# Attention and two feed-forward layers on one core: raw keys and queries of two heads transposed side by side, reciprocals spread through DRAM, a written order per tile

## The reference

```
def _attn_ref(q, k, v):                       # q, k, v: 4 x 8 heads x 1152 x 64
    q_pool = q.reshape(B, H, S // 2, 2, D).mean(axis=3)
    scores = scale * np.matmul(q_pool, k.transpose(0, 1, 3, 2))
    scores = scores - np.max(scores, axis=-1, keepdims=True)
    attn = np.exp(scores)
    attn = attn / (np.sum(attn, axis=-1, keepdims=True) + 1e-09)
    return np.matmul(attn, v)

# x = attention's output as 2304 tokens x 512
h = x @ w_in                                  # 512 x 2048
x = np.where(h >= 1, h, np.where(h <= -1, 0, (h + 1) ** 2 / 4)) @ w_out
x = np.maximum(np.maximum(x @ w1, x @ w2), x @ w3) @ w2_out      # 512 x 768, 768 x 512
```

## Time and profile before

| | us |
|---|---|
| runs | 1294.75, 1292.39, 1293.17 |
| median | 1293.17 |
| the profiled execution's own time | 1294.91 |
| its span, first to last instruction | 1293.0 |
| PE busy in the span | 1259.6 (97%) |
| DVE, ACT, POOL busy | 758.1, 658.8, 335.5 |

### The profile page before, as it was taken

One profiled execution on the slowest core, in us unless ns is written; L12 is line 12 of the kernel. 1 busy time (PEld: TensorE's weight loads), 2 busy tenths in 40 slices (PEclk: granted clock), 3 DMA queues, 4 the chain that ended last, 5 costly groups with the idle time before them and its releaser, 6 DMA issues.

```text
span 1293.0 us, 21136 instructions
## 1 busy us (share of the span) xinstructions
PE 1259.6 (97%) x7876; PEld 1207.9 (93%) x7876; DVE 758.1 (59%) x1579; ACT 658.8 (51%) x1570; POOL 335.5 (26%) x332
## 2 busy tenths in 40 slices
PE   7999999999999999989999999999999999999998
PEld 6989899999989898979999999999999999999997
DVE  5888888888888888874544444444453222223221
ACT  5989899999989898962222222222222111111111
POOL 5343443444433444258600000000282000000000
PEclk9999999999999999989999999999999999999999
DMA  3111111111111111113300000000030000000000
GB/s 119 47 56 56 52 33 57 53 41 56 56 47 56 56 56 38 52 49 100 113 1 1 1 1 1 1 1 1 17 122 26 1 25 25 1 25 5 20 25 25
DMA packets 59140, 49.07 MB, mean 38 GB/s; under 512 B 2977, under 2 KB 48033, under 8 KB 59041
## 3 DMA queue, kind: packets, MB, share of 16 engines
q1 hardware_dynamic: 59040, 47.72, 12.1%
HBM read 42.99 MB, written 4.72 MB: 37 GB/s over the span
## 4 chain that ended last, share of the span: by engine, by line
PE 79%; ACT 18%; DVE 1%; issue 1%; POOL 1%; DMA 0%; SPq 0%; POOLq 0%; ACTq 0%
PE hid L868 33%; PE acc L900 16%; ACT probs L558 8%; PE trans L413 8%; ACT pT_hi L548 6%; PE acc L932 6%; PE scores L456 6%; PE values L475 5%; PE scores L458 4%; ACT kT L568 1%; ACT value_aux L582 1%; PE trans L424 1%; DVE qT L662 1%; ACT X L578 1%; ACT qT L571 1%
## 5 line engine op out<-in xcount | busy, mean ns | idle before, releaser
L626 DVE TENSOR_REDUCE neg_max_parts<-scores 128x1 f32<-128x384 f32 x432 | 234.7, 552 | 44.0 <-PE scores L458 30.3
L548 ACT ACTIVATE pT_hi<-trans 128x384 fp32r<-128x384 f32 x432 | 191.2, 491 | 55.8 <-PE trans L413 52.3
L640 DVE TENSOR_TENSOR pT_lo<-trans,pT_hi 128x384 fp32r<-128x384 f32 x432 | 212.0, 546 | 7.3 <-ACT pT_hi L548 6.3
L558 ACT ACTIVATE probs<-scores,neg_max 128x768 f32<-128x768 f32 (+1 forms) x288 | 212.0, 753 | 4.0 <-DVE neg_max L633 4.0
L456 PE MATMUL scores<-kT,qT 128*128 128x384 f32 x480 | 199.6, 416 | 9.4 <-ACT probs L558 9.1
L413 PE MATMUL trans<-ident,probs 128*128 128x128 f32 x1296 | 189.7, 273 | 9.6 <-DVE qT L662 6.4
L413 PEld LDWEIGHTS trans<-ident,probs 128*128 128x128 f32 x1296 | 157.5, 140 | 24.9 <-DVE qT L662 11.5
L868 PE MATMUL hid<-qT,w_slots 128*128 128x384 f32 x936 | 171.6, 336 | 0.0
L868 PE MATMUL hid<-x_hi,w_slots 128*128 128x384 f32 x624 | 167.6, 335 | 0.0
L868 PEld LDWEIGHTS hid<-qT,w_slots 128*128 128x128 f32 x936 | 163.7, 188 | 1.0
L986 ACT ACTIVATE excess<-rise,halves 128x384 f32<-128x384 f32 x96 | 59.2, 617 | 203.0 <-DVE rise L1070 203.0
(11 more groups left out here) (101 smaller groups left out, 1998.2 us busy)
## 6 DMA issues: line engine op xcount, KB each, us to landing
k_raw<-in_k SPq DMA_DIRECT2D x16, 576.0 KB, 4.0
v_raw<-in_v SPq DMA_DIRECT2D x32, 288.0 KB, 2.8
q_raw<-in_q SPq DMA_DIRECT2D x32, 256.0 KB, 3.0
out<-X SPq DMA_DIRECT2D x18, 256.0 KB, 2.8
q_raw<-in_moe_w_out SPq DMA_DIRECT2D x14, 256.0 KB, 3.1
k_raw<-in_moe_w SPq DMA_DIRECT2D x12, 256.0 KB, 3.1
k_raw<-in_moe_w_in SPq DMA_DIRECT2D x8, 256.0 KB, 2.9
k_raw<-in_moe_w_out SPq DMA_DIRECT2D x8, 256.0 KB, 3.0
```

The costliest lines, as they stand in the source:

```text
L548: act.activation(*tile_places(pT[0], src, t, g), ACT.Copy).then_inc(p_hi_done, 1)
L558: act.activation(probs[:, par, :].rearrange("p (n k) -> p n k", n=GROUPS)[:, ns[0]:ns[-1] + 1], scores[:, bank:bank + len(ns), 0:SB], ACT. ...
L626: dve.tensor_reduce(neg_max_parts[:, par, n:n + 1], scores[:, score_banks(u9)[n], 0:SB], AX_X, ALU.max, negate=True).then_inc(parts_done, 1)
L640: dve.tensor_tensor(*tile_places(pT[1], src, t, g), hi.bitcast(F32), ALU.subtract).then_inc(p_lo_done, 1)
```

## The change

Keys: `load_k` writes two heads side by side (runs of 64 elements), PE transposes the raw keys, 9 blocks in three groups, ACT writes the high part (`k_hi_done`), DVE the remainder (`k_lo_done`), both into `k_parts`, and SP places them in `kT` with four copies of 64 partitions. Queries: POOL adds the neighbours so that two heads stand side by side, PE transposes 4 blocks and one for the shared tile, ACT and DVE write `q_parts`, SP places them with eight copies. Values: ACT keeps a whole block with one instruction, SP moves the other head's half under its partner (`move_values`), POOL adds. Reciprocals: SP writes the 128x9 to DRAM (4-byte runs), reads them back with three broadcasts into `recip_cols`, and POOL multiplies all of a pair's `X` (`scale`). The first pair keeps the old layout; its keys are split by DVE as before, after both new loads. The order strings now differ from tile to tile. At the end POOL splits eight weight chunks early, the high part of the first `X` tile is written by ACT, and no transposes of reciprocals stand between the first products.

```
-PREP = {0: [("K", 0)], 1: [("K", 1)], 2: [("K", 2)], 3: [("K", 3)], 4: [("K", 4), ("R", 0)],
-        5: [("K", 5)], 6: [("R", 1), ("Q", 0), ("Q", 1), ("Q", 2)]}
-PE_ORDER = ["S1", "T0", "S2", "T1", "T2", "N0", "V", "X"]
-ACT_ORDER = ["T0", "T1", "T2", "E0", "E1", "X", "V"]
-DVE_ORDER = ["T0", "T1", "T2", "M0", "X", "M1", "M2"]
+PE_ORDER = """
+S1.1 S1.2
+T0.0 T0.1 S2.0 W2:10-14 K0 T0.2 W2:14-18 S2.1 S2.2
+T1.0 T1.1 T1.2 S3.0 W3:0-4 W3:4-8 K1 S3.1 W3:8-10 S3.2
+T2.0 T2.1 S4.0 T2.2 K2 S4.1
+T3.0 S4.2 T3.1 W3:10-13 S5.0 T3.2 W3:13-15 Q0 S5.1 W3:15-18
+T4.0 S5.2 T4.1 V0:0-4 S6.0 T4.2 V0:4-8 S6.1 S6.2
+T5.0 Q1 V0:8-13 S7.0 V0:13-18 T5.1 S7.1 S7.2 T5.2
+T6.0 S8.0 T6.1 V1:0-4 T6.2 V1:4-8 S8.1 S8.2
+T7.0 T7.1 V1:8-13 T7.2 V1:13-18
+T8.0 S9.0 S9.1 S9.2 T8.1 T8.2 S10.0 V2:0-5 V2:5-10
+"""
...
-    KG, QG, RG = 6, 3, 2
+    KG, QG = 3, 2
...
-            sp.dma_start(k_raw, k_heads[bass.ds(head(pair), 2)].rearrange("h p n -> p h n")
-                         ).then_inc(k_loaded, 16)
+            for h in range(2):
+                src = k_heads[bass.ds(head(pair) + h, 1)].rearrange("h p (t d) -> p (h t) d", d=D)
+                sp.dma_start(k_raw[:, :, h, :], src).then_inc(k_loaded, 16)
...
+        def place_k(pair):
+
+            sp.wait_ge(k_lo_done, pair * KG)
+            for h in range(2):
+                for a in range(2):
+                    copy_parts(sp, kT[rows_of(a), pair % 2, h, :], k_parts[rows_of(h), a, :], k_placed)
+
+        def place_q(pair):
+
+            sp.wait_ge(q_lo_done, (pair - 1) * QG + 1)
+            for part, dst in enumerate((qT_hi, qT_lo)):
+                for h in range(2):
+                    at = (2 + 4 * h) * P
+                    for copy in range(2):
+                        copy_parts(sp, dst[rows_of(copy), pair % 2, at:at + 4 * P], q_parts[rows_of(h), part, :], q_placed)
...
+        def scale(pair):
+
+            pool.wait_ge(recip_spread, 48 * (pair + 1))
...
+            x = X[:, bass.ds(pair * SQ, SQ)]
+            pool.tensor_tensor(x, x, recip_cols[:], ALU.mult).then_inc(scaled, 1)
...
-    EARLY = 3
+    EARLY, EARLY_LOADS = 8, 5
...
+        if n == 0:
+            pool.wait_ge(*ends["keys_placed"])
+        elif n == 1:
+            pool.wait_ge(*ends["scores_done"])
+        elif n == 2:
+            pool.wait_ge(*ends["values_done"])
+        split_weights(pool, n, n)
```

More of the change, by code:

```diff
@@ L144, in prep_of, with ring_order @@
-    def prep_of(u, t, first, last):
-        return [(kind, g) for kind, g in PREP.get(t, [])
-                if not (kind == "R" and first and u == 0) and not (kind in "KQ" and last and u == 1)]
-    def group_count(kind, pair, t, g):
+    WARM_UP, BRIDGE = 22, 10
+    FIRST = [("FK", 0), ("FK", 1), ("FK", 2), ("FQ", 0)]
+    SECOND = [("FK", 3), ("FK", 4), ("FK", 5), ("FQ", 1), ("FQ", 2)]
+    def ring_order():
+        groups = FIRST + SECOND
+        for pair in range(PAIRS):
+            for step in steps_of(PE_ORDER):
+                if step[0] == "T":
+                    groups.append(("T", pair * TILES + step[1], step[2]))
+                elif step[0] in "KQ" and pair + 1 < PAIRS:
+                    groups.append((step[0], pair + 1, step[1]))
+        return groups
@@ L289, in sp_program @@
[L289 to L316 removed]
+        load_v(0, 0)
@@ L437, in tile_scores @@
[L437 to L443 removed]
+                last = pe.transpose(trans[:, BANK[group], j * P:(j + 1) * P], probs[:, s % 2, at:at + P], ident[:])
+            last.then_inc(tile_trans_done, 1)
@@ L874, in hidden1 @@
         idx = tile * C1 + f
+        if idx == 0:
+            pe.wait_ge(*ends["exp_done"])
         if f == 0:
@@ L942, in two_tiles1 @@
                 for f in range(C1):
-                    if not (first and u == 0 and f < EARLY):
-                        hidden1(pe, tile, f, u)
+                    hidden1(pe, tile, f, u)
                     if f >= LAG1:
```

955 lines of the change are left out of this document (478 added, 477 removed).

## The result

The changed kernel takes 1311.7 us (median of 4 runs, 1308.6 to 1315.6), the kernel before 1292.85 beside it: a ratio of 1.0145, interval 1.0132 to 1.0159. It is slower where 1250 was forecast. The profiled execution has a span of 1313.9 us against 1293.0. From the page of the changed kernel: the span, busy time of PE, granted clock and DMA share in forty slices, packets, and the load queue.

What follows compares the result with a forecast made beforehand. PE was taken as the bound, ACT and DVE close behind. From 1294.9 us, 40.3 off for 15.5 attention pairs at 32.2 us, 2 added at the start, 6 off at attention's end: 1250.6, stated as 1250, range 1231 to 1271.

Runs made afterwards that it cites:

- e1: The changed kernel with the reciprocals stored as 128 runs of 36 bytes instead of 1152 single 4-byte numbers (output wrongly scaled): 1271.96 us.
- e4: The changed kernel with the reciprocals transposed by PE, copied by ACT and stored as 9 runs of 512 bytes behind the second move: 1277.02 us.
- e5: e4 with SP's next keys' load moved from behind the keys' copies to behind the queries' copies: 1270.01 us.
- e2: The changed kernel with SP issuing the eight queries' copies right behind the four keys' copies, scattered store kept: 1324.76 us.
- e8: The changed kernel with the same scattered store of reciprocals issued by ACT into its own DMA queue instead of by SP: 1332.65 us.
- e9: The changed kernel with the scattered store issued behind the values' load and second move, and at the end a move right behind it: 1319.31 us.

## What to carry to other kernels

Price every transfer that a change adds by how its writes lie in DRAM, not by its bytes: a scattered store of touching 4-byte numbers cost 40 us (the changed kernel against e1), and one small transpose ahead of it took 35 of them back (e4), with a load moved in SP's order 42 (e5). Look then at what stands behind it in every queue, since reads of DRAM wait for it wherever they were issued. And before a transfer is moved forward, look which buffer the overtaken ones give back, and who needs it (e2: 13 us lost by the "obvious" cure).

## What the hardware did that I had not expected

Numbers of 4 bytes, 1152 of them: complete in 10.4 us when they touch, 6.6 with 8 bytes from one to the next, 4.0 with 32 or 64 (each of the last three with a small store ahead of it). I have not shown what unit of memory they contend for. The hold crosses queues (e8), and it grows in proportion (10.4, 19.7 for two). Data copied inside SBUF passes it for the most part (77 ns a packet at 607 us; in e9's body 225 of 3840 packets over 1 us), its completion does not (marks at 612.8 to 615.2). A copy of 4608-byte runs from 64 partitions to 64 others inside SBUF took 326 ns a packet in the changed kernel, against 93 for 2304 bytes from DRAM, both medians: 14 against 25 bytes a ns.
